# A recurrent attention stage with one decay scan a pair and its inverse summed on TensorE, and a last stage worked in quads

## The chip, the core and the metric

The kernel runs on one core of a Trainium2 chip. The metric is device time in microseconds (us), from one launch to its end. The core's engines are TensorE (PE, with its weight loads as PEld), VectorE (DVE), ScalarE (ACT), GpSimd (POOL) and SyncE (SP), which here only issues DMAs. TensorE's clock is granted at one of two levels, 2.4 GHz (1.00 in the profile) or 1.2 GHz (0.50).

## What is computed

A linear recurrent attention over 4 batches x 8 heads, 768 steps, 40 dimensions a head, then a top-2 mixture of experts (8 experts, 3072 tokens, 320 -> 1024 -> 320), then a feed-forward layer with the gate h * tanh(softplus(h)). All inputs are float32.

```python
for t in range(S):
    y[:, :, t] = np.einsum('bhd,bhde->bhe', rt, state)
    Sa = np.einsum('bhde,bhe->bhd', state, at)
    state_decay = state * wt[:, :, None, :] - np.einsum('bhd,bhe->bhde', Sa, bt)
    state = state_decay + np.einsum('bhd,bhe->bhde', vt, kt)
...
for e in range(E):
    for k in range(2):
        mask = top2[:, k] == e
        h = np.maximum(x[mask] @ w1[e], 0.0)
        out[mask] += top2_w[mask, k, None] * (h @ w2[e])
...
h = x @ w_in
sp = np.where(h > 20.0, h, np.log1p(np.exp(np.minimum(h, 20.0))))
return ((h * np.tanh(sp)) @ w_out).astype(np.float32)
```

## The kernel before

Four stages follow each other: attention, routing (`route`), the expert tiles (`experts`), and the last feed-forward layer (`mish_ffn`). The change touches the first and the last.

**Attention.** The 768 steps are cut into 12 chunks (NC) of 64 (C), two halves of 6 chunks (HC). The 32 heads are 16 pairs; a group holds two pairs (i = 0, 1), so there are 8 groups (GR). A pair's two heads lie in partitions 0 to 63 and 64 to 127. Within a chunk the recurrence is solved in closed form: the decays are folded into `a`, `b` and `k`; N and T are the strictly triangular products of `a` with `b`, and the inverse of one minus N is built by squaring: `npow` and `tpow` hold the powers 2, 4, 8, 16 (steps n2 to n16, t2 to t8), and `wb` the running sum (steps w2 to w16). Steps L, E and F refine it once in float32. Other steps are M, G, K, B, V (products that don't need the state), and UT, ST, H, J, Y, X, which form the output of a half. Each of these steps, called "wide", is one call of `wide(tok, g)` on TensorE: 24 or 48 small matmuls into one of three PSUM buffers `wide0` to `wide2`, which ScalarE or VectorE (`take`) empties. `BY_ACT` names those that ScalarE empties. The step's buffer is reused three steps later, so TensorE waits for that.

The state itself passes from chunk to chunk in a chain of "hops" in PSUM tile `chain`: `u` (ScalarE copies it to `un`), `s` (VectorE updates `st`) and `r` (VectorE adds to `rhs`), 34 hops a group.

What sets the order is the written table `ORDER`. Every engine walks through it once an iteration, 10 iterations (GR + 2) in all: in one iteration stand the wide steps of group g, the chain of group g - 1 with the first-half output steps, and the second-half output steps of group g - 2. `p0` and `p1` are VectorE's `make_decays` for the next group. SP loads the inputs of the next group at fixed places of the table (decays and `a` at its start, `kbv` and `r` when G1 is filled), and POOL scales `a`, `k`, `b` with the decays (`scale_a`, `scale_kb`), for which N0 of the next group waits.

The decays of a chunk are cumulative products. Before, each pair takes two scans over 768 columns, one forwards (`dec`) and one backwards (`after`), a ratio `fend` and a reciprocal of 12 columns; the state is carried divided by decays, and `s` adds with a scalar per chunk, `fs` being the scaled old state that VectorE prepares behind each `r`.

Ahead of all this POOL sets the padded input tiles, after which SP may load; VectorE clears tiles and makes masks; ScalarE issues one DMA that zeroes `slots` (9 MB) for the routing stage.

**Last stage** (`mish_ffn`). Its 24 row tiles are worked in 6 groups of 4 (GT); the 16 column blocks of the hidden layer (FT) each take three matmuls of 512 columns over 128, 96 and 96 input rows (`KT`). ScalarE runs exp block by block, then ln and tanh for a whole group at once; VectorE caps and copies each hidden block out of PSUM and multiplies (`gate`) the group before. `rows_out` of a group stands behind the next group's hidden blocks.

## Time and profile before

| | us |
|---|---|
| time, median of 3 runs | 1853.9 (1849.0 to 1856.9) |
| the profiled execution, its own time | 1852.9 |
| its span | 1851.0 |
| attention: TensorE's first matmul, its last | 47.0, 683.2 |
| busy in the span: TensorE, its weight loads | 1526.4, 1211.4 |
| busy in the span: VectorE, ScalarE, POOL | 600.5, 469.2, 296.9 |
| mean granted clock of TensorE | 0.864 |

The profile is of one execution. Its views are: the page (shares, 40 slices, chain, groups), the groups of instructions by line, the waits (who waited for whom), the DMA queues, the timeline, and stretches ("windows") with the busy time of each engine and the granted clock. "Idle ... <- X" names what ended an engine's idle time; "issue" is time in which it waited for nothing that the profile shows. An engine's busy time is not its bound: what counts is what ends last in each stage.

### The profile page before, as it was taken

To read this page: it belongs to the slowest core of one execution; us is meant where nothing else is said; L and a number is where in the kernel's file an instruction comes from. 1 tells how busy PE (TensorE), PEld (TensorE's weight loads), DVE (VectorE), ACT (ScalarE), POOL (GpSimd) and SP (SyncE) were. 2 spreads that over 40 slices of the span, in tenths; PEclk is the share of its full clock that TensorE was granted. 3 is DMA by queue.
4 is the path that set the end of the run, shared out by engine and by line. 5 is a ranking of instruction groups with operands and counts; after the bars stand their busy time and mean duration, and the time that the engine had idled before them with its cause. 6 is when DMAs were issued, how large, how long until landed. Compare 5 with 4: busy or idle time off the path is not lost. (4 is left out here: it accounts for less than half of the span.)

```text
span 1851.0 us, 52932 instructions
## 1 busy us (share of the span) xinstructions
PE 1526.4 (82%) x23913; PEld 1211.4 (65%) x23913; DVE 600.5 (32%) x1176; ACT 469.2 (25%) x845; POOL 296.9 (16%) x273
## 2 busy tenths in 40 slices
PE   0778777777778769009999999999959999999999
PEld 0777677777777659008888888888834555565556
DVE  5554545545454311300000000000015625526251
ACT  0322323223233211001111111111103635243340
POOL 6413212132221000450000000000031100100000
PEclk9667877787777855559999999999979999999999
DMA  7412111221110019236555555555351100100000
GB/s 260 134 36 69 52 52 54 72 77 52 52 52 25 10 37 295 78 140 211 170 170 175 177 178 178 177 175 174 117 160 49 29 23 28 29 22 0 15 7 22
DMA packets 98652, 177.36 MB, mean 96 GB/s; under 512 B 37280, under 2 KB 66720, under 8 KB 97152
## 3 DMA queue, kind: packets, MB, share of 16 engines
q1 hardware_dynamic: 84128, 140.23, 24.8%
q0 software_dynamic: 7248, 24.75, 4.0%
q10 hardware_dynamic: 7056, 9.01, 1.4%
q8 instruction: 191, 3.13, 0.7%
q14 instruction: 29, 0.24, 0.0%
HBM read 140.20 MB, written 33.75 MB: 94 GB/s over the span
## 5 line engine op out<-in xcount | busy, mean ns | idle before, releaser
L1071 PE MATMUL mpH<-mxT,win 96*128 96x512 f32 (+1 forms) x576 | 253.4, 596 | 2.2 <-ACT mxT L1107 2.2
L948 PE MATMUL pY<-down,hT 128*128 x880 | 245.9, 433 | 0.0
L929 PEld LDWEIGHTS pH<-exT,up 128*128 128x128 f32 x1760 | 207.8, 194 | 15.0 <-DMA up_rest<-in_moe_w 4.9
L929 PE MATMUL pH<-exT,up 128*128 128x128 f32 x1760 | 208.3, 277 | 5.9 <-DMA up_rest<-in_moe_w 4.4
L984 DVE COPY ys<-pY 128x320 f32<-128x320 f32 x55 | 27.1, 492 | 570.6 <-PE pY L948 570.6
L1080 PE MATMUL mpY<-wout,h 128*128 128x320 f32 x768 | 207.5, 432 | 0.0
L948 PEld LDWEIGHTS pY<-down,hT 128*128 128x128 f32 x880 | 163.0, 190 | 61.2
L1071 PEld LDWEIGHTS mpH<-mxT,win 96*128 96x128 f32 (+1 forms) x576 | 108.4, 191 | 133.3 <-issue 129.8
L1080 PEld LDWEIGHTS mpY<-wout,h 128*128 128x128 f32 x768 | 145.6, 190 | 60.5 <-issue 0.5
L975 ACT ACTIVATE hT<-pH 128x512 f32<-128x512 f32 x110 | 59.7, 594 | 422.6 <-PE pH L934 422.6
L1115 ACT ACTIVATE act_in<-act_in 128x512 f32<-128x512 f32 x96 | 59.9, 629 | 243.1 <-DVE act_in L1157 243.1
L908 POOL DMA_DIRECT2D results<-ys x55 | 29.8, 541 | 509.4 <-DVE ys L984 509.4
L482 ACT ACTIVATE npow<-wide 128x768 bf16<-128x768 f32 x80 | 64.8, 810 | 160.5 <-PE wide L298 135.4
L1157 DVE TENSOR_SCALAR act_in<-mpH 128x512 f32<-128x512 f32 x96 | 66.3, 691 | 83.7 <-PE mpH L1071 82.4
L918 PE MATMUL pX<-ident,xs 128*128 128x128 f32 x110 | 24.4, 304 | 74.6 <-DMA xs<-slots 74.6
L1050 POOL DMA_INDIRECT rows<-results,pos x48 | 46.7, 973 | 221.5 <-DVE mix L1133 205.8
L268 POOL TENSOR_TENSOR kbvT<-kbvT,after 128x768 f32<-128x768 f32 x32 | 57.4, 1825 | 93.9 <-DMA kbvT<-in_kbv 93.9
L1138 DVE COPY y<-mpY 128x320 f32<-128x320 f32 x24 | 11.8, 492 | 174.5 <-PE mpY L1080 168.3
L1158 DVE COPY h<-mpH 128x512 f32<-128x512 f32 x96 | 65.5, 682 | 0.0
L918 PEld LDWEIGHTS pX<-ident,xs 128*128 128x128 f32 x110 | 11.2, 142 | 81.6 <-DMA xs<-slots 75.1
L934 PE MATMUL pH<-exT,up_rest 64*128 64x128 f32 x880 | 63.9, 285 | 0.0
L449 PE MATMUL chain<-rhs,w 64*64 64x40 f32 x768 | 50.2, 261 | 16.3 <-DVE rhs L591 14.7
(173 smaller groups left out, 2304.3 us busy)
## 6 DMA issues: line engine op xcount, KB each, us to landing
up<-in_moe_w SPq DMA_DIRECT2D x55, 1024.0 KB, 5.3
up_rest<-in_moe_w SPq DMA_DIRECT2D x110, 128.0 KB, 5.2
kbvT<-in_kbv SPq DMA_DIRECT2D x32, 360.0 KB
down<-in_moe_w SPq DMA_DIRECT2D x8, 1280.0 KB, 14.2
slots<-zero_row ACTq DMA_DIRECT2D x1, 8800.0 KB, 48.1
xs<-slots SPq DMA_DIRECT2D x55, 160.0 KB, 5.1
results<-ys POOLq DMA_DIRECT2D x55, 160.0 KB, 2.1
wfr<-in_wdec SPq DMA_DIRECT2D x32, 240.0 KB
```

The source lines that it names most:

```text
L268: nc.gpsimd.tensor_tensor(kbvT[i][:, j, :], kbvT[i][:, j, :], after[i][:, ::-1], ALU.mult).then_inc(kb_scaled, 1)
L449: m = pe.matmul(chain[x:x + 64, i, 64:64 + D], w0[b2][x:x + 64, i, cols(c, C)], rhs[b2][x:x + 64, i, c, :], start=(c == 0), stop=True, ski ...
L482: return nc.scalar.activation(out, in_, ACT.Copy, scale=scale)
L929: pe.matmul(pH[t % 2][b][:, c, :], up[t % NU][:, k, f * P:(f + 1) * P], xT[t % 2][:, k, :], start=(c == 0 and k == 0), stop=False, skip_gr ...
L934: m = pe.matmul(pH[t % 2][b][:, c, :], up_rest[t % NU][at, c * P:(c + 1) * P], xT[t % 2][at, 2, :], start=False, stop=True, skip_group_che ...
L948: m = pe.matmul(pY[t % 2][:, 0:D], hT[t % 2][:, j, :], down[:, bass.ds(e, 1), j, :].rearrange("q n d -> q (n d)"), start=(j == 0), stop=(j ...
L975: nc.scalar.activation(hT[t % 2][:, b * HT:(b + 1) * HT, :], pH[t % 2][b][:], ACT.Relu).then_inc(h_copied[b], 1)
L1071: m = pe.matmul(pH[n % 4][:], win[0:kn, k, f * P:(f + 1) * P], xT[g % 2][0:kn, k, :], start=(k == 0), stop=(k == 2))
L1080: m = pe.matmul(pY[t % 2][:, 0:D], h[g % 2][:, f, j * P:(j + 1) * P], wout[:, f, :], start=(f == 0), stop=(f == FT - 1))
L1115: nc.scalar.activation(act_in[g % 2][:, f, :], act_in[g % 2][:, f, :], ACT.Exp).then_inc(exped, 1)
L1157: nc.vector.tensor_scalar(act_in[g % 2][:, f, :], pH[n % 4][:], 20.0, None, ALU.min).then_inc(h_min, 1)
L1158: nc.vector.tensor_copy(h[g % 2][:, f, :], pH[n % 4][:]).then_inc(h_used, 1)
```

## The change

In attention:
- `make_decays` is one scan over 12 x 65 columns (`dec`, with the decay at the end of a chunk in column 64) and one reciprocal of 768 columns (`rec`), which scales `k` and `b`.
- The state is carried unscaled: an `s` hop adds (`total`) and then multiplies by the chunk's decay (`past`); `fs` is gone.
- For the odd pair (i = 1) the powers, the running sum, L, E and F alternate between straight and swapped halves (`turned`, `flips`), so that both pairs together use all four quarters; ST and J likewise, for which `r` of the odd pair is loaded a second time (`rTo`).
- The running sum is formed in PSUM: each `w` step gets 24 more matmuls with the identity (`plus=wb`); ScalarE then copies w2, w4, w8, VectorE copies w16.
- E adds the identity on VectorE, and POOL subtracts it from `n32` ahead of time (before, POOL prepared `wm` behind w16).
- `ORDER` is a new table.
- At the start VectorE sets `wtok`; SP loads the decays behind that, `r` and `v` next, then `a` and `kbv`, each behind its own memset; the zeroing of `slots` waits for `kbv` and uses rows of 640 bytes.

In the last stage a quad (four column blocks) is the unit: eight matmuls over 128 rows, then four over 64 rows that stand alternately in the lower and upper half (`win_rest`); exp, ln and tanh follow in each quad, `act_in` has three buffers, and the turn of a row tile and `rows_out` of one row tile stand behind each quad.

```diff
-ORDER = """N0 u UT1 s N1 ST1 r T0 u H1 T1 s M0 r J1 u Y1 s M1 r n2_0 u t2_0 K s n2_1 p0 r t2_1 B u X1 p1 s G0 r n4_0 t4_0 u
-G1 s n4_1 t4_1 w2_0 r V0 u w2_1 n8_0 s t8_0 w4_0 r V1 u n8_1 t8_1 s w4_1 UT0 r n16_0 w8_0 u ST0 n16_1 s w8_1 H0 r
+ORDER = """N0 u UT1 s N1 r T0 ST1 u H1 t2_0 s T1 J1 r Y1 u n2_0 s n2_1 w2_0 r M1 u n4_0 w2_1 s M0 w4_0 r p0 B u t2_1 V1
+s n4_1 t4_0 r G0 u UT0 s t8_0 w4_1 r n8_0 u V0 n16_0 p1 t4_1 s K ST0 r G1 u w8_0 n8_1 s t8_1 r u w8_1 n16_1
...
-BY_ACT = ("n2", "n4", "n8", "n16", "t2", "t4", "t8", "K", "B", "V", "L", "UT", "ST", "X")
+BY_ACT = ("n2", "n4", "n8", "n16", "t2", "t4", "t8", "w2", "w4", "w8", "K", "B", "V", "L", "UT", "ST", "X")
...
+        def turned(i, x, flip):
+
+            return 64 - x if flip and i else x
...
-            sp.wait_ge(pads_set, 1)
+            sp.wait_ge(w_pads, 1)
             load_decays(0)
-            load_a(0)
-            load_kbv(0)
             load_r(0)
             load_v(0)
+            sp.wait_ge(pads_set, 1)
+            load_a(0)
+            sp.wait_ge(pads_set, 2)
+            load_kbv(0)
+            sp.wait_ge(pads_set, 3)
...
-            def square(b, g, half, out, left, right):
+            def square(half, out, left, right, flips, plus=None):
+
                 for c in range(HC):
                     k = half * HC + c
                     for i, h, e, x in cells():
-                        m = pe.matmul(out[x:x + 64, i, cols(c, C)], left[x:x + 64, i, cols(k, C)], right[x:x + 64, i, cols(k, C)],
-                                      start=True, stop=True)
+                        q, z = turned(i, x, flips[0]), turned(i, x, flips[1])
+                        m = pe.matmul(out[z:z + 64, i, cols(c, C)], left[q:q + 64, i, cols(k, C)], right[q:q + 64, i, cols(k, C)],
+                                      start=True, stop=plus is None)
+                    if plus is not None:
+                        for i, h, e, x in cells():
+                            q, z = turned(i, x, flips[0]), turned(i, x, flips[1])
+                            m = pe.matmul(out[z:z + 64, i, cols(c, C)], identh[q:q + 64, q:q + 64], plus[q:q + 64, i, cols(k, C)],
+                                          start=False, stop=True)
                 return m
...
-                        if p == 1:
-                            m.then_inc(carried, 1)
+                        for i, h, e, x in cells():
+                            r = rTo[b3][x:x + D, cols(k, C)] if i else rT[b3][x:x + D, 0, cols(k, C)]
+                            pe.matmul(out[e:e + D, i, cols(c, C)], sm[x:x + D, i, k, :], r, start=(k in (1, HC)), stop=False, skip_group_check=True)
...
-                after_step(nc.vector.tensor_tensor_scan(after[i][:], wfr[i][:, 1, :], mark_r[:], 0.0, ALU.mult, ALU.add))
-                after_step(nc.vector.tensor_tensor(fend[:, g % 3, i, :], after[i][:, ::-1][:, 0::C], wfr[i][:, 0, 1::C], ALU.mult))
-                after_step(nc.vector.reciprocal(mark[:, 0::C], fend[:, g % 3, i, :]))
-                nc.vector.tensor_tensor_scan(dec[g % 3][i][:], wfr[i][:, 0, :], mark[:], 0.0, ALU.mult, ALU.add).then_inc(decayed, 1)
+                after_step(nc.vector.tensor_tensor_scan(dec[g % 3][:, i].rearrange("q c f -> q (c f)"), wtok[i][:].rearrange("q c f -> q (c f)"),
+                                                        mark[:].rearrange("q c f -> q (c f)"), 0.0, ALU.mult, ALU.add))
+                nc.vector.reciprocal(rec[i][:], dec[g % 3][:, i, :, 1:C + 1]).then_inc(decayed, 1)
...
-                    nc.vector.scalar_tensor_tensor(st[:, 1, c + 1, :], chain[:, 1, 128:128 + D], fend[:, g % 3, 1, c + 1:c + 2], fs[:, 1, :],
-                                                   ALU.mult, ALU.add).then_inc(state_ready, 1)
+                    nc.vector.tensor_tensor(total[:], chain[:, :, 128:128 + D], st[:, :, c, :], ALU.add).then_inc(summed, 1)
+                    dve.wait_ge(summed, (NC - 2) * g + c)
+                    nc.vector.tensor_tensor(st[:, :, c + 1, :], total[:], past, ALU.mult).then_inc(state_ready, 1)
...
-                for k, (k0, kn) in enumerate(KT):
-                    m = pe.matmul(pH[n % 4][:], win[0:kn, k, f * P:(f + 1) * P], xT[g % 2][0:kn, k, :], start=(k == 0), stop=(k == 2))
-                m.then_inc(h_done, 1)
...
+                for f in range(GT * q, GT * q + GT):
+                    wait(pe, h_used, g * FT + f - 3)
+                    for k in range(2):
+                        pe.matmul(pH[f % 4][:], win[:, k, f * P:(f + 1) * P], xT[g % 2][:, k, :], start=(k == 0), stop=False)
+                for f in range(GT * q, GT * q + GT):
+                    at = slice(f % 2 * REST, (f % 2 + 1) * REST)
+                    pe.matmul(pH[f % 4][:], win_rest[at, f // 2 * P:(f // 2 + 1) * P], xT[g % 2][at, 2, :],
+                              start=False, stop=True).then_inc(h_done, 1)
...
+                for late in ((), (0,), (1,), (2, 3))[n] if n < GT else (n,):
+                    gate(late)
```

Three places of the instruction order follow. First VectorE in attention, around the decays of pair 0 of the next group (`p0`). `mT` is step M, `rhs` an `r` hop, `st` an `s` hop. Before:

```order
L555 TENSOR_TENSOR mT<-wide0,mask_u 128x2x384
L591 TENSOR_TENSOR rhs0<-chain,rhs0 128x2x40
L593 TENSOR_TENSOR fs<-st,fend 128x80
L599 SCALAR_TENSOR_TENSOR st<-chain,fend,fs 128x40
L601 SCALAR_TENSOR_TENSOR st<-chain,fend,fs 128x40
L581 SCALAR_TENSOR_TENSOR after0<-wfr0,mark_r 128x768
L582 TENSOR_TENSOR fend<-after0,wfr0 128x12
L583 RECIPROCAL mark<-fend 128x12
L584 SCALAR_TENSOR_TENSOR dec2_0<-wfr0,mark 128x768
```

And after the change:

```order
L572 TENSOR_TENSOR mT<-wide0,mask_u 128x2x384
L605 TENSOR_TENSOR rhs0<-chain,rhs0 128x2x40
L596 SCALAR_TENSOR_TENSOR dec2<-wtok0,mark 128x780
L598 RECIPROCAL rec0<-dec2 128x768
L611 TENSOR_TENSOR total<-chain,st 128x80
L613 TENSOR_TENSOR st<-total,dec0 128x2x40
L605 TENSOR_TENSOR rhs0<-chain,rhs0 128x2x40
L572 TENSOR_TENSOR gT1<-wide1,mask_u 128x2x384
```

The decays stood behind an `s` hop's state update and ahead of an `r` hop's addition; they now stand behind an addition and ahead of a state update.

Second TensorE in the last stage, a turn, hidden blocks (`mpH`) and output rows (`mpY`). Before:

```order
L1071 MATMUL mpH0<-mxT1,win 128x512 x3
L1071 MATMUL mpH1<-mxT1,win 128x512 x3
L1071 MATMUL mpH2<-mxT1,win 128x512 x3
L1071 MATMUL mpH3<-mxT1,win 128x512 x3
L1060 MATMUL mpX1<-ident,mix1 128x128
L1060 MATMUL mpX1<-ident,mix1 96x128 x2
L1080 MATMUL mpY0<-wout,h0 128x320 x16
L1080 MATMUL mpY1<-wout,h0 128x320 x16
```

And after:

```order
L1095 MATMUL mpH0<-mxT1,win 128x512 x2
L1095 MATMUL mpH1<-mxT1,win 128x512 x2
L1095 MATMUL mpH2<-mxT1,win 128x512 x2
L1095 MATMUL mpH3<-mxT1,win 128x512 x2
L1098 MATMUL mpH0<-mxT1,win_rest 128x512
L1098 MATMUL mpH1<-mxT1,win_rest 128x512
L1098 MATMUL mpH2<-mxT1,win_rest 128x512
L1098 MATMUL mpH3<-mxT1,win_rest 128x512
L1083 MATMUL mpX0<-ident,mix0 128x128 x3
L1108 MATMUL mpY0<-wout,h0 128x320 x16
```

A block had three matmuls in a row; now four blocks have two each and their third ones stand together, and one row tile's output follows each quad.

Third ScalarE in the last stage, at the end of a group before:

```order
L1115 ACTIVATE act_in<-act_in 128x512 x4
L1106 ACTIVATE mxT<-mpX 128x128
L1107 ACTIVATE mxT<-mpX 96x2x128
L1120 ACT_TABLE_LOAD
L1120 ACTIVATE act_in<-act_in 128x2048 x4
L1123 ACT_TABLE_LOAD
L1123 ACTIVATE act_in<-act_in 128x2048 x4
```

And in every quad after:

```order
L1145 ACTIVATE act_in<-act_in 128x512 x4
L1137 ACTIVATE mxT<-mpX 128x3x128
L1149 ACT_TABLE_LOAD
L1149 ACTIVATE act_in<-act_in 128x2048
L1151 ACT_TABLE_LOAD
L1151 ACTIVATE act_in<-act_in 128x2048
```

Two table loads a group of 16 blocks have become two a quad of four.

## Rows read from the trace of the kernel before

**Rows 1.** Stretches, us: busy (count) PE, PEld, DVE, ACT, POOL; clock, DMA.

```profile
101.00:560.00 459.00, 350.58 (x13716) 333.17 (x13716) 239.39 (x453) 138.17 (x249) 115.61 (x72) 0.76 0.20 58
...
1388.00:1851.00 463.00, 458.57 (x1399) 259.06 (x1397) 208.35 (x352) 171.43 (x196) 31.47 (x32) 1.00 0.07 23
```

**Rows 2.** Waits of PE, 47 to 690 us: us in total, times, longest.

```profile
PE wide L298 <- issue: 32.0, 17, 5.0
PE chain L437 <- DVE st L601: 21.4, 27, 3.2
PE chain L449 <- DVE rhs L591: 14.7, 28, 1.2
...
PE wide L328 <- issue: 0.2, 1, 0.2
```

**Rows 3.** DMA queues, 110 to 560 us, then 580 to 638: packets, MB, share.

```profile
q8 instruction: 106, 1.74, 1.6%
...
q8 instruction: 15, 0.25, 1.9%
```

**Rows 4.** Timeline of TensorE, 286 to 297 us: start us, us, engine, line, operation.

```profile
289.48 0.55 PE L298 MATMUL wide<-wb,npow 64*64 64x64 bf16 x24
289.86 0.55 PE L298 MATMUL wide<-npow,tpow 64*64 64x64 bf16 x24
...
295.51 0.32 PE L298 MATMUL wide<-wb,npow 64*64 64x64 bf16 x5 [3.96 <-issue]
```

**Rows 5.** Groups by line and form: busy us, mean ns of one, idle before.

```profile
L407 PE MATMUL wide<-rT,sm 40*40 40x64 f32 x704 | 36.1, 284 | 0.8 <-issue 0.8
...
L298 PE MATMUL wide<-w,n 64*64 64x64 f32 x768 | 26.9, 226 | 0.0
...
L398 PE MATMUL wide<-rT,unT 40*64 40x64 f32 x768 | 22.0, 264 | 10.2 <-issue 10.2
```

**Rows 6.** Timeline of all engines, 0 to 60 us.

```profile
15.36 3.77 SPq L179 DMA_DIRECT2D wfr<-in_wdec  x4
...
26.77 1.76 DVE L581 TENSOR_TENSOR_SCAN after<-wfr,mark_r 128x768 f32<-128x768 f32 x1 [17.37 <-DMA wfr<-in_wdec]
...
34.38 1.76 DVE L584 TENSOR_TENSOR_SCAN dec<-wfr,mark 128x768 f32<-128x768 f32 x1
...
38.14 7.53 POOL L268 TENSOR_TENSOR kbvT<-kbvT,after 128x768 f32<-128x768 f32 x4
...
47.04 2.84 PE L320 MATMUL wide<-kbvT,aT 40*64 40x64 f32 x96 [47.04 <-DVE mask_un L621]
```

**Rows 7.** Groups by line and form: VectorE's two reciprocals.

```profile
L583 DVE RECIPROCAL mark<-fend 128x12 f32<-128x12 f32 x16 | 3.7, 230 | 0.6
...
L814 DVE RECIPROCAL gates<-gap 128x24 f32<-128x24 f32 x1 | 0.3, 303 | 0.0
```

**Rows 8.** The chain that ended last, in the last stage: start us, us.

```profile
1506.88 10.31 PE mpH L1071 x24
1517.19 0.33 PE mpX L1060 x3
```

**Rows 9.** Timeline of TensorE in the expert stage, 1000 to 1014 us.

```profile
1002.46 3.73 PE L929 MATMUL pH<-exT,up 128*128 128x128 f32 x32
1006.12 1.16 PE L934 MATMUL pH<-exT,up_rest 64*128 64x128 f32 x16
1007.22 0.44 PE L918 MATMUL pX<-ident,xs 128*128 128x128 f32 x2
```

**Rows 10.** Groups by line and form in the last stage: VectorE's, then ScalarE's.

```profile
L1157 DVE TENSOR_SCALAR act_in<-mpH 128x512 f32<-128x512 f32 x96 | 66.3, 691 | 83.7 <-PE mpH L1071 82.4
...
L1115 ACT ACTIVATE act_in<-act_in 128x512 f32<-128x512 f32 x96 | 59.9, 629 | 243.1 <-DVE act_in L1157 243.1
...
L1120 ACT ACTIVATE act_in<-act_in 128x2048 f32<-128x2048 f32 x24 | 43.9, 1897 | 0.1
...
L1120 ACT ACT_TABLE_LOAD x6 | 7.7, 1283 | 0.1
```

More of the change, by code:

```diff
@@ L112, in attention @@
         rT = [sb(f"rT{b}", [P, 2, S]) for b in range(3)]
+        rTo = [sb(f"rTo{b}", [P, S]) for b in range(3)]
         vtok = [sb(f"vtok{b}", [P, 2, NC, D]) for b in range(2)]
@@ L194, in load_r @@
                         sp.dma_start(rT[g % 3][64 * h:64 * h + D, i, :], rt[2 * g + i, h]).then_inc(r_loaded, 16)
+                for h in range(2):
+                    sp.dma_start(rTo[g % 3][64 * (1 - h):64 * (1 - h) + D, :], rt[2 * g + 1, h]).then_inc(r_loaded, 16)
             def load_v(g):
@@ L350, in wide @@
                     left, right = (tpow, npow) if kind[0] == "n" else (npow, tpow)
-                    m = square(b2, g, half, out, left[at_], right[at_])
+                    m = square(half, out, left[at_], right[at_], {2: (0, 0), 4: (0, 1), 8: (1, 0), 16: (0, 1)}[p])
                 elif kind[0] == "w":
@@ L358, in wide @@
                         taken(pe, f"w{p // 2}_{half}", g)
-                    m = square(b2, g, half, out, npow[(p.bit_length() + 1) % 2], wb)
+                    m = square(half, out, npow[(p.bit_length() + 1) % 2], wb, (0, 1) if p in (2, 8) else (1, 0), plus=wb)
                 elif kind == "L":
@@ L364, in wide @@
                         for i, h, e, x in cells():
-                            m = pe.matmul(out[x:x + 64, i, cols(c, C)], wb[x:x + 64, i, cols(k, C)], identh[x:x + 64, x:x + 64], start=True, stop=True)
+                            z = turned(i, x, 1)
+                            m = pe.matmul(out[z:z + 64, i, cols(c, C)], wb[x:x + 64, i, cols(k, C)], identh[x:x + 64, x:x + 64], start=True, stop=True)
                 elif kind == "E":
                     taken(pe, f"w16_{half}", g)
-                    m = square(b2, g, half, out, n32, w0[b2])
+                    pe.wait_ge(less, 2 * g + half + 1)
+                    m = square(half, out, n32, w0[b2], (0, 1))
                 elif kind == "F":
@@ L371, in wide @@
                     taken(pe, f"E{half}", g)
-                    m = square(b2, g, half, out, npow[1], tpow[1])
+                    m = square(half, out, npow[1], tpow[1], (1, 0))
                 elif kind == "UT":
@@ L391, in wide @@
                         for i, h, e, x in cells():
-                            m = pe.matmul(out[e:e + D, i, cols(c, D)], st[e:e + D, i, k, :], ident[e:e + D, e:e + D], start=True, stop=True)
+                            m = pe.matmul(out[x:x + D, i, cols(c, D)], st[e:e + D, i, k, :], ident[e:e + D, e:e + D], start=True, stop=True)
                 elif kind == "H":
@@ L993, in mish_ffn @@
     G = N // P // GT
+    FQ = FT // GT
+    REST = D - 2 * P
     with ExitStack() as ctx:
@@ L1058, in turn, with hidden @@
                 wait(pe, copied, t - 1)
-                for k, (k0, kn) in enumerate(KT):
-                    m = pe.transpose(pX[t % 2][0:kn, k, :], mix[t % 2][:, k0:k0 + kn], ident[:])
+                for k in range(3):
+                    m = pe.transpose(pX[t % 2][:, k, :], mix[t % 2][:, k * P:(k + 1) * P], ident[:])
                 m.then_inc(turned, 1)
-            def hidden(g, f):
-                if f == 0:
+            def hidden(n):
+                g, q = divmod(n, FQ)
+                if q == 0:
@@ L1080, in rows_out @@
+            def rows_out(t, fs):
+                g, j = divmod(t, GT)
+                if fs.start == 0:
+                    wait(pe, y_copied, t - 1)
+                for f in fs:
+                    if j < 2 and f % GT == 0:
+                        pe.wait_ge(gated, g * FT + f + GT)
                     m = pe.matmul(pY[t % 2][:, 0:D], h[g % 2][:, f, j * P:(j + 1) * P], wout[:, f, :], start=(f == 0), stop=(f == FT - 1))
-                m.then_inc(y_done, 1)
+                if fs.stop == FT:
+                    m.then_inc(y_done, 1)
@@ L1083, in _ @@
             for t in range(GT):
                 turn(t)
-            for g in range(G):
-                for f in range(FT):
-                    hidden(g, f)
-                    if f % 4 == 3 and g + 1 < G:
-                        turn((g + 1) * GT + f // 4)
-                if g == 1:
-                    pe.wait_ge(wout_loaded, 16)
-                if g > 0:
-                    for j in range(GT):
-                        rows_out(g - 1, j)
-            for j in range(GT):
-                rows_out(G - 1, j)
+            for n in range(G * FQ):
+                hidden(n)
+                if n + GT < G * GT:
+                    turn(n + GT)
+                if n == GT:
+                    pe.wait_ge(wout_loaded, 16)
+                if n >= GT:
+                    rows_out(n - GT, range(FT))
@@ L1098, in _ @@
+            first = (G - 1) * GT
+            for fs in (range(FT - GT), range(FT - GT, FT)):
+                for t in (first, first + 1):
+                    rows_out(t, fs)
+            for t in (first + 2, first + 3):
+                rows_out(t, range(FT))
         @block.scalar
```

241 lines of the change are left out of this document (110 added, 131 removed).

## The prediction

> **What bounds the kernel now.** I read the profile in this order: stretches of the span with their granted clock, what TensorE waits for, the DMA queues, then single stretches of the timeline.
>
> The stretches say which stage is bound by what. In the last stage, from 1388 us on, TensorE is busy 458.6 of 463 us at clock 1.00 [rows 1]: what it has to stream is the time. In the middle of attention, 101 to 560 us, it is busy 350.6 of 459 us at a mean clock of 0.76, which is 1.2 GHz for half of the time and 2.4 for the other half [rows 1]; the other 108 us are waits. The largest are put down to "issue", TensorE waiting for nothing that the profile shows: thirteen such rows from the first to the last, 91.7 us together. Waits for VectorE come behind: 21.4 us for `st` and 14.7 us for `rhs` [rows 2].
>
> "Issue" is the supply of instructions. Between 110 and 560 us the instruction queue brings 106 packets of 16.4 KB, one per 4.25 us [rows 3]. In about that stretch TensorE executes 2 x 13716 instructions [rows 1], so a packet holds some 254 of them. Where no group's inputs are loaded (580 to 638 us) it is still one packet per 3.87 us [rows 3]. And TensorE stops inside one helper call in which nothing is waited for: 3.96 us before five matmuls of a square, while 24 such matmuls take 0.38 us at full clock (289.48 to 289.86) [rows 4]. So in attention an instruction costs what its share of a packet costs, whatever it computes, unless it streams longer than that.
>
> **The change part by part**, against the profiled execution (1852.93 us, span 1851.0; the median of the three runs is 1.0 us above it).
>
> *Inverse summed on TensorE.* Each of the eight `w` steps of a group gets 24 identity matmuls: 8 x 8 x 24 = 1536, with their weight loads 3072 instructions, 12.1 packets, at 3.87 us: +47 us. Bounds: at 24 in 0.38 us with the supply free, +24 us; at 4.25 us a packet, +51 us. I take the quiet packet, since the bursts of input loads don't multiply. The additions that VectorE loses are not on the path; the copies go to ScalarE, which idles in attention.
> The Trainium skill ("Runtime: NRT & Kernel Launch", Instruction fetch mechanics) says that fetching is hidden, since instructions are dispatched more slowly than the blocks are filled. The stops of 3.96 us within a call speak against it here. By it the sum would have +24 us for this step.
>
> *Odd pair on swapped halves.* Before, steps J (L407) and E (L298 on `w`, `n`, f32) use only two of the four quarters of the array: J costs 36.1/704 = 51 ns a matmul record, E 26.9/768 = 35 ns, while the same form on all four quarters costs 22.0/768 = 28.6 ns [rows 5]. Now both use all four: 704 x 22.7 = 16 us and 768 x 6.4 = 5 us, together -21 us (bounds: nothing, where the supply paces them anyway, and -21). The bf16 squares stream 64 columns in 0.38/24 = 16 ns at full clock [rows 4], under the supply's 3.87/128 = 30 ns a record, so four quarters give them nothing.
>
> *One decay scan a pair.* The two scans, the ratio and the small reciprocal (9.4 us for two pairs, 26.77 to 36.14 [rows 6]) become one scan of 1.8 us and a reciprocal of 768 elements a row. No row shows such a one. 12 elements take 230 ns and 24 take 303 ns [rows 7], 6.1 ns an element: 230 + 756 x 6.1 = 4.8 us. Bounds: an element-wise operation (691 ns for 512 [rows 10]) gives 1.0 us; 303/24 for each element gives 9.7 us. I take 4.8, on the slope of the only two rows. The block is then 6.6 us, which cannot be interrupted, twice an iteration; behind it on VectorE stands the state update, for which the next `r` hop waits.
> The cover: from `rhs` to that `r` hop the new order puts B, a `u` hop, t2_1, V1, the `s` hop, n4_1 and t4_0, some 240 records, 8 us at 33 ns (4.25/128). The second block has n8_0, u, V0, n16_0, t4_1, s, K and ST0, 280 records, 9 us. Block and state update (7.2 us) fit in both: no cost, as long as the reciprocal stays under about 5.6 us.
>
> *Unscaled state.* An `s` hop has two dependent operations where two independent ones stood, and the rescaling behind `r` is gone. Only where the chain runs alone, eleven chunks at the end, does it count: +1 us.
>
> *New order.* VectorE has 144 fewer rows, and dependent steps stand further apart. TensorE's two largest waits for VectorE sum to 36 us [rows 2]; I take not quite a quarter off: -8 us; bounds -25 and +25, since the order can as well put two late producers in a row. G1 moves behind the second block, and SP issues the loads of `kbv` and `r` behind G1. There remain some 820 records, 27 us, for the load (1.4 MB; 9 us is my estimate) and POOL's scaling (7.5 us [rows 6]): hidden, with 10 us to spare.
>
> *Start.* Before: SP issues the first load at 15.36 us, behind all of POOL's memsets, VectorE starts at 26.77, has both pairs at 36.14, and the masks, slowed while POOL scales, take until 47.04 [rows 6]. Now SP waits for two memsets of VectorE, about 2.7 us, and the zeroing of `slots` no longer competes. The decays land before VectorE has done its other memsets (about 10 us); two blocks end at 23.2; the same 10.9 us for masks give 34. So -13 us. Bounds by the reciprocal: 1.0 us gives -20, 9.7 us -3. The zeroing now runs behind the first loads, over POOL's and VectorE's preparation and the first steps of TensorE; before, it reached some 10 us into them as well: 0.
>
> *Last stage.* Four column blocks cost 10.31 us in 24 records of 0.43 us [rows 8]. Now 16 full records (6.87 us) and four pairs of half-height records. The expert stage shows such pairs: sixteen records of 128 columns take 1.10 us (1006.12 to 1007.22 [rows 9]), where eight full ones take 0.93 (3.73 us for 32). So they do run side by side, and going in and out costs 0.17 us. 6.87 + 4 x 0.43 + 0.17 = 8.76 us: -1.55 x 24 = -37 us.
> Something is late behind it. While no output rows are due, TensorE needs 9.1 us a quad (8.76 and 0.33 for the transposes [rows 8]). ScalarE needs 4 x 0.63, a copy of about 0.5, 2 x 1.90 and now two table loads of 1.28 a quad [rows 10]: 9.4 us. Its first quad is done 12.3 us after the first hidden block (VectorE's 3 x 1.38 + 0.69, then one exp, the copy, and both loads and long operations), its fourth at 12.3 + 3 x 9.4 = 40.5; VectorE then gates it (4 x 0.69) and only then mixes the rows that the turn behind the fifth quad needs (about 1.2 us, an estimate), at 44.5. TensorE is there at 4 x 9.1 + 0.9 = 37.3: +7 us, once (bounds 0 and +10). Later a quad has 17 us of TensorE, and VectorE's loop (12.3 + 2.8 + 1.2 + 0.5 = 16.8) fits. Net -30 us.
>
> **Sum:** +47 - 21 + 0 + 1 - 8 - 13 - 30 = -24 us: 1852.9 - 24 = 1829 us.
>
> **The rivals.**
> *A, the supply does not pace it.* Then the identities cost 24 us instead of 47, and the bf16 squares gain from four quarters at the low clock, where a record of 64 columns takes 53 ns and two at a time make 27 a record: a few ns of each of some 4200, about 10 us. 1829 - 23 - 10 = 1796 us. For it: at the low clock TensorE hardly stops. Against: 92 us of stops. It is what the Trainium skill's section on instruction fetch (in "Runtime: NRT & Kernel Launch") would lead to. Its chance is 0.25.
> *B, the reciprocal is uncovered (slower).* Place: the blocks on VectorE ahead of the state update. Price at 9.7 us: a block and update of 12.1 us against covers of 8 and 9 us, 7 us an iteration, 7 iterations, 49 us, and 10 us at the start: 1888 us. It turns the whole to slower from a reciprocal of about 8 us on. Against: the slope of [rows 7]. Chance 0.1.
> The Trainium skill ("VectorE: DVE Perf Modes", the 8-slice pipeline) has the divide repeat 8 times an element; at its 0.96 GHz that is an estimate of 6.4 us, which costs about 9 us here by the same working.
> *C, the gains of attention don't come.* J and E are paced by the supply already (+21), a packet costs 4.25 us (+4) and the new order wins no waits (+8): 1862 us. Chance 0.17.
> *D, the change doesn't do what it says:* records of 512 columns don't pair in the last stage, +37: 1866 us. Against: [rows 9]. Chance 0.04.
> The forecast has 0.44.
>
> **How the numbers follow.** A measurement can tell about 0.5%, 9 us, from no change. Under 1844.6 us lie most of the forecast (0.37), A, and a little of C: 0.65. Within lie the rest of the forecast and most of C: 0.18. Above lie B, D and the tail of C: 0.17. The range 1790 to 1866 holds the forecast, A and most of C and leaves out B.
>
> **What would show it.** TensorE's first matmul at 34 us; RECIPROCAL of 768 elements at 4.8 us; 203 instruction packets, an iteration of attention 1 to 3 us longer than before; J and E under 30 ns a record; quads of 8.76 us; one wait of some 7 us for `mix` behind the fifth quad; a last stage of about 435 us. Wrong would be: fewer "issue" waits with as many packets (A), `st` waits of several us twice an iteration (B), a long wait of N0 for POOL's scaling, or rows in the last stage of 10.3 us a quad (D).

## The result, and the profile after

The changed kernel takes 1870.4 us (median of 5 runs, 1863.6 to 1873.0) where the kernel before takes 1853.9 (1849.0 to 1856.9). The ratio is 1.0088, with a 95% interval of [1.0062, 1.0114]: 16 us slower. The forecast was 1829 us, with a range of 1790 to 1866: the change went the other way, and the time lies outside the range. The profiled execution has a span of 1869.0 us, 18.0 more than before.

The starts and ends of TensorE's work in the two traces (us) give the place:

| | before | after | changed by | forecast |
|---|---|---|---|---|
| first matmul | 47.04 | 36.86 | -10.2 | -13 |
| attention, first to last matmul | 636.2 | 692.9 | +56.7 | +19 |
| routing and experts, up to VectorE's last copy of results | 673.1 | 673.0 | -0.2 | 0 |
| last stage, first hidden block to last matmul | 465.1 | 437.7 | -27.4 | -30 |

The start and the last stage came nearly as forecast. Attention lost three times what was forecast.

The profile's page of the changed kernel: the clock granted to TensorE in 40 slices, and the DMA queues (packets, MB, share).

```profile
PEclk9996666657765766555999999999997999999999
...
q10 hardware_dynamic: 14096, 9.01, 1.6%
q8 instruction: 203, 3.33, 0.8%
```

The 203 instruction packets are the number forecast. Next, TensorE's waits in the changed kernel from 30 to 700 us (engine, tile and line, what was waited for: us in total, times, longest), the answer to [rows 2]:

```profile
PE wide L310 <- issue: 53.6, 36, 5.9
...
PE wide L336 <- ACT xr L495: 27.8, 5, 6.2
PE chain L450 <- DVE st L613: 16.5, 23, 1.6
PE wide L336 <- issue: 15.6, 11, 2.7
...
PE chain L462 <- DVE rhs L605: 5.2, 14, 1.1
```

The waits for VectorE fell from 21.4 and 14.7 us to 16.5 and 5.2, and "issue" rose (all its rows: 135 us, where 92 stood). The row of `xr` was not in the trace of before at all: step N (L336 in the changed kernel) waits five times, up to 6.2 us, for ScalarE's copy into `xr`, the attention output on its way to memory.

One of the five, in the timeline of all engines around 427 us (start us, us, engine, line, operation; in brackets the idle time ahead):

```profile
426.07 0.43 PE L462 MATMUL chain<-rhs,w 64*64 64x40 f32 x8
426.59 0.83 SPq L204 DMA_DIRECT2D vtok<-in_vtok  x2
427.47 5.22 SPq L210 DMA_DIRECT2D x_by_pair<-xr  x4
431.13 0.63 ACT L495 ACTIVATE xr<-wide 128x240 f32<-128x240 f32 x2 [8.69 <-DMA x_by_pair<-xr]
...
431.81 1.56 PE L336 MATMUL wide<-kbvT,aT 40*64 40x64 f32 x48 [5.31 <-ACT xr L495]
```

Read it from the end. TensorE's N0 cannot start before 431.81, because it reuses the PSUM buffer of X0, and ScalarE copies X0 out only from 431.13 on. ScalarE was idle for 8.69 us, since it copies into `xr` only when the earlier stores from it have landed. SP issued the last of these at 427.47, behind the load of `v`, and that load stands behind a wait for the last `u` hop, 426.07. So the last hop of an iteration, a load, a store, its landing, a copy and the first step of the next iteration became one chain. Before, the store stood ahead of the loads of `kbv`.

### The profile page after: what moved, and what is told of

Read it like the earlier page. It is cut to its first block and busy times, and to the rows that moved or that the text cites. A ratio compares the mean times of both kernels' runs of the same rounds, so it can differ in the third digit from the quotient of the medians.

```text
span 1869.0 us, 55904 instructions
## 1 busy us (share of the span) xinstructions
PE 1492.0 (80%) x25449; PEld 1180.2 (63%) x25449; DVE 607.3 (32%) x1041; ACT 554.8 (30%) x905; POOL 284.3 (15%) x268
## 5 line engine op out<-in xcount | busy, mean ns | idle before, releaser
L1095 PE MATMUL mpH<-mxT,win 128*128 128x512 f32 x384 | 173.3, 605 | 4.9 <-ACT mxT L1137 4.7
L1095 PEld LDWEIGHTS mpH<-mxT,win 128*128 128x128 f32 x384 | 74.1, 194 | 92.2 <-issue 82.8
L1175 DVE TENSOR_TENSOR h<-h,act_in 128x512 f32<-128x512 f32 x96 | 59.9, 686 | 142.8 <-ACT act_in L1151 142.7
L310 PE MATMUL wide<-wb,npow 64*64 64x64 bf16 x1536 | 60.3, 234 | 26.3 <-issue 23.0
L598 DVE RECIPROCAL rec<-dec 128x768 f32<-128x768 f32 x16 | 79.2, 4953 | 0.5
L336 PE MATMUL wide<-kbvT,aT 40*64 40x64 f32 x768 | 24.3, 300 | 64.7 <-DVE mask_un L635 36.9
L275 POOL TENSOR_TENSOR kbvT<-kbvT,rec 128x768 f32<-128x768 f32 x32 | 57.4, 1826 | 93.8 <-DMA kbvT<-in_kbv 93.8
L495 ACT ACTIVATE un<-chain 128x80 f32<-128x80 f32 x96 | 22.9, 238 | 163.9 <-PE chain L462 163.7
```

The source lines that it names most:

```text
L275: nc.gpsimd.tensor_tensor(kbvT[i][:, j, :], kbvT[i][:, j, :], rec[i][:].rearrange("q c f -> q (c f)"), ALU.mult).then_inc(kb_scaled, 1)
L310: m = pe.matmul(out[z:z + 64, i, cols(c, C)], left[q:q + 64, i, cols(k, C)], right[q:q + 64, i, cols(k, C)], start=True, stop=plus is None)
L495: return nc.scalar.activation(out, in_, ACT.Copy, scale=scale)
L598: nc.vector.reciprocal(rec[i][:], dec[g % 3][:, i, :, 1:C + 1]).then_inc(decayed, 1)
L1095: pe.matmul(pH[f % 4][:], win[:, k, f * P:(f + 1) * P], xT[g % 2][:, k, :], start=(k == 0), stop=False)
L1175: nc.vector.tensor_tensor(at, at, act_in[n % 3][:, f, :], ALU.mult).then_inc(gated, 1)
```

## The experiments

Ratios are to the kernel before, measured beside each, with 95% intervals; 0.1% is 1.85 us. Differences between two kernels are taken between their ratios. Lines in a trace move by one or more with each edit.

**1. The store ahead of the wait.** In the changed kernel the store of the second half goes ahead of the wait for the last hop (not back to its old place ahead of `kbv`, since X1 comes late in the new order):

```diff
                     sp.wait_ge(filled, number["V1", it] + 1)
+                if it >= 2:
+                    store(it - 2, 1)
+                if g < GR:
                     if it >= 1:
                         sp.wait_ge(hopped, it * HOPS)
                     load_v(g)
-                if it >= 2:
-                    store(it - 2, 1)
```

> The changed kernel with one edit: SP issues the store of the second half of x (group it-2) ahead of its wait for the last hop and ahead of the load of v, not behind them. Theory S (the moved store): ScalarE's copy of x for the first half waits for that store to land, and the next N step of TensorE waits for that copy, 27.8 us in five waits of the changed kernel's trace, one for each iteration that both loads and stores. They go: 1870 - 28 = 1842 us, no wait of TensorE on xr over 1 us, an iteration of attention about 5.6 us shorter. Rival I (instruction supply): attention's 57 us come from instructions; packets go on arriving at one per 4.2 us and the waits on xr turn into waits put down to issue: 1862 to 1870 us.

Measured: 0.9960 [0.9925, 0.9994]; the same kernel measured again (experiment 3), 0.9969 [0.9946, 0.9993]. That is 22 to 24 us faster than the changed kernel, and attention takes 668.6 us in the trace instead of 692.9. The row of waits for `xr` is gone. SP's store now follows a copy into `xr` at once (timeline, 400 to 417 us):

```profile
404.94 0.61 ACT L496 ACTIVATE xr<-wide 128x240 f32<-128x240 f32 x2
405.62 1.93 SPq L210 DMA_DIRECT2D x_by_pair<-xr  x2
```

Theory S holds. The other way round, the same edit was made alone in the kernel before:

```diff
-                if it >= 2:
-                    store(it - 2, 1)
...
                     load_v(g)
+                if it >= 2:
+                    store(it - 2, 1)
```

> The kernel before with only SP's store of the second half moved behind the load of v, as in the changed kernel. Theory S: the copy of x for the first half then waits for a store that is issued only behind the last hop, and F1, which reuses its buffer, waits for the copy: five times about 5.6 us, 1854 + 28 = 1882 us. Rival I: the wait is an effect of the new order alone, and here the store has slack: 1854 to 1858 us.

Measured: 1.0094 [1.0059, 1.0129], 17 us slower. Its waits show the new row, in the place where it was expected:

```profile
PE wide L298 <- ACT xr L482: 27.3, 5, 6.0
```

27.3 us of waits cost 17 to 19 us (attention is 19.2 us longer, 655.4). The expectation of 28 took each wait at its full length, but some of it had stood elsewhere before: in the traces TensorE's "issue" waits in attention fell from 91.8 to 84.8 us.

**2. The identities.** The early-store kernel (that of experiment 1) first without them, so that the running sum is left out, and then with all of them at an eighth of their columns, so that most of the sum is left out:

```diff
-m = square(half, out, npow[(p.bit_length() + 1) % 2], wb, (0, 1) if p in (2, 8) else (1, 0), plus=wb)
+m = square(half, out, npow[(p.bit_length() + 1) % 2], wb, (0, 1) if p in (2, 8) else (1, 0))
```

> The previous kernel (early store) without the 1536 identity matmuls of the eight w steps: the sum with the old w is left out of the computation, nothing takes its place. Supply theory of the prediction: 3072 instructions fewer, 12 packets at 3.9 us: 47 us less than the kernel with them. Rival A of the prediction (the supply does not pace it, an instruction costs its streaming): 24 us less. A third: the time is set by waits between engines and the identities stand in their shade, under 15 us less.

Measured: 0.9759 [0.9700, 0.9817]: 37 us less than with them by the ratios, 43 by the medians, 45 in attention's time in the traces (623.4 for 668.6 us). It is the +47 of the forecast, a little less. The two intervals together allow some 12 us either way, so that the 24 of rival A lies at their edge; experiment 6, which does the sum without identities, gains 45 us with 10 either way and leaves it out.

```diff
-m = pe.matmul(out[z:z + 64, i, cols(c, C)], identh[q:q + 64, q:q + 64], plus[q:q + 64, i, cols(k, C)],
+m = pe.matmul(out[z:z + 64, i, c * C:c * C + 8], identh[q:q + 64, q:q + 64], plus[q:q + 64, i, k * C:k * C + 8],
...
```

> The kernel with the early store, with all 1536 identity matmuls in place, each adding 8 of its 64 columns only (the rest of the sum is left out). Supply theory: the instruction count sets the time, 1845 us as with 64 columns. Work theory (rival A): 56 of 64 columns less at 10 to 19 ns a record, about 20 us less, 1825 us or below.

Measured: 0.9951 [0.9923, 0.9978], 2 to 3 us less than with 64 columns, which the intervals cannot tell from none. The pages have the same packets in the kernel with 8 columns, and 12 fewer without the identities:

```profile
q8 instruction: 203, 3.33, 0.7%
```

```profile
q8 instruction: 191, 3.13, 0.7%
```

So an identity costs because it is an instruction, and hardly for what it streams. Where a packet comes each 3.87 us ([rows 3]), twelve are 46 us.

The short identities alone can't tell the supply from a fixed cost of each matmul on TensorE itself: with 8 columns as with 64 an identity starts on average 13.6 ns behind the matmul ahead of it (gaps of 200 ns and more left out). But 1536 times 13.6 ns are 21 us, half of what the identities cost, and without them TensorE's "issue" waits in attention fall from 140.1 to 116.1 us. Experiment 3 is the other half of the argument: there work is taken away and no instruction, and nothing is gained.

The Trainium skill ("Runtime: NRT & Kernel Launch", Instruction fetch mechanics) has fetching hidden behind the dispatch of instructions; in this stage, with 64-column matmuls, these runs speak against it.

**3. Four quarters instead of two.** The early-store kernel, with J as in the kernel before (e5), with the squares, E, F and L in one place (e6), and with both (e14). The core of the edits:

```diff
-            return 64 - x if flip and i else x
+            return x
...
-r = rTo[b3][x:x + D, cols(k, C)] if i else rT[b3][x:x + D, 0, cols(k, C)]
-pe.matmul(out[e:e + D, i, cols(c, C)], sm[x:x + D, i, k, :], r,
+m = pe.matmul(out[e:e + D, i, cols(c, C)], sm[e:e + D, i, k, :], rT[b3][e:e + D, i, cols(k, C)],
...
```

> The kernel with the early store, but step J again on two quarters of TensorE's array, pair 1 first and pair 0 behind it, as in the kernel before (the extra rows of r are still loaded). The prediction's term: 704 records from 28.6 to 51 ns, 16 us more than 1845. If the supply paces J either way, as the small gain of the whole suggests: 0 to 5 us more.

> The kernel with the early store, but every step that the change put on swapped halves except J (the squares n, t, w with their identities, L, E and F) on two quarters again. The prediction's term: E 5 us, bf16 squares nothing: 5 us more. By the record rates in the two traces (bf16 squares 26 and 14 ns a record where the clock is low) up to 30 us more. If the supply paces all: 0.

Measured: 0.9979 [0.9943, 1.0014] and 0.9936 [0.9909, 0.9963]; against 0.9960 that is 3.5 us more and 4.4 us less, both inside the intervals. To settle it, both edits together and the kernel without them were measured side by side:

> The kernel with the early store, with J and the squares, E, F and L all on two quarters of the array: the change without its swapped halves. The prediction's terms J and E are 21 us: 1866 us. From the two single runs (J +4, the squares -5, both within their intervals): 1840 to 1850 us, no difference from the same kernel on four quarters in this call.

> The kernel with the early store again, as the mate of the one on two quarters in this call: 1845 us.

Measured: 0.9964 [0.9942, 0.9986] on two quarters, 0.9969 [0.9946, 0.9993] on four (medians 1844.1 and 1844.3 us). Together the swapped halves are worth nothing; 21 us lie outside what the two intervals allow (about 6 us either way). Yet the edit does what it says. Busy time of the engines from 101 to 560 us, as in [rows 1], first on two quarters, then on four:

```profile
101.00:560.00 459.00, 361.11 (x14139) 346.04 (x14136) 235.80 (x314) 159.39 (x269) 106.37 (x68) 0.73 0.17 50
```

```profile
101.00:560.00 459.00, 337.33 (x14200) 316.57 (x14204) 233.88 (x315) 160.24 (x273) 106.52 (x68) 0.67 0.18 53
```

TensorE gets through as many matmuls in the stretch (14139 and 14200). On four quarters it is busy 23.8 us less for them, and this at a lower mean clock; it stands idle for what it saved. "Issue" waits of the whole stage are 143 us where the other kernel has 128. It looks as if a faster step only reached the next missing instruction earlier; the runs show the idle time, not its cause. (Over the whole of attention the two profiled executions are 10 us apart, 669.8 us on four quarters and 680.0 on two, but the profiled execution on two quarters was the slowest of its twelve, 1858.4 us; the ratios show no difference.)

**4. The order.** The early-store kernel with the table `ORDER` of the kernel before, then the kernel before with the new table (its store of the second half moved ahead of the wait for the last hop, as in experiment 1, because X1 comes late in the new order):

```diff
-ORDER = """N0 u UT1 s N1 r T0 ST1 u H1 t2_0 s T1 J1 r Y1 u n2_0 s n2_1 w2_0 r M1 u n4_0 w2_1 s M0 w4_0 r p0 B u t2_1 V1
+ORDER = """N0 u UT1 s N1 ST1 r T0 u H1 T1 s M0 r J1 u Y1 s M1 r n2_0 u t2_0 K s n2_1 p0 r t2_1 B u X1 p1 s G0 r n4_0 t4_0 u
...
```

> The kernel with the early store in the order of steps of the kernel before. The prediction has the new order at 8 us (bounds -25 and +25): 8 us more than 1845. Rival: the new order gains nothing or loses, since dependent steps of a square now wait in it less but producers are late in a row: 1845 or less.

> The kernel before in the new order of steps, with the store of x's second half issued ahead of the wait for the last hop (in the new order that half is ready only late in the iteration). The prediction gives the new order 8 us, bounds -25 and +25: 1852 - 8 = 1844 us. If the order is worth in the kernel before what it is worth in the changed one (37 to 49 us), 1805 to 1815 us. If it serves only to cover the new, longer decay block, 1852 us or more.

Measured: 1.0187 [1.0141, 1.0234] for the old order in the changed kernel, 42 us more than the new; 0.9951 [0.9933, 0.9969] for the new order in the kernel before, 9 us less than before, the 8 us of the forecast. The two numbers differ because the decay block has changed. With the old order, the early-store kernel waits for `st`, at most 5.7 us at a time:

```profile
PE chain L451 <- DVE st L614: 46.7, 32, 5.7
```

The old order has a block right ahead of an `r` hop (`p0`) and right ahead of an `s` hop (`p1`), whose additions VectorE then makes late. In the new order VectorE can start a block as soon as it has done an `r` hop's addition, and a `u` hop and three wide steps or more (B, t2_1 and V1; n8_0, V0, n16_0 and t4_1) come ahead of the `s` hop whose state it must update next. The trace tells the block from the unscaled state, whose two dependent operations are new as well: with the old order a scan or reciprocal of the decays ran during 16 of TensorE's waits for `st` and `rhs`, 44.4 us together; in the early-store kernel this happens in two waits, 0.4 us. How much of the cover is used up shows with the reciprocal computed twice:

```diff
+                after_step(nc.vector.reciprocal(rec[i][:], dec[g % 3][:, i, :, 1:C + 1]))
                 nc.vector.reciprocal(rec[i][:], dec[g % 3][:, i, :, 1:C + 1]).then_inc(decayed, 1)
```

> The kernel with the early store, with each reciprocal of the decays computed twice, one behind the other: a block on VectorE takes 1.8 + 2 x 4.95 = 11.7 us and not 6.8. By the prediction's covers of 8 and 9 us (its rival B: 59 us at 9.7 us more than it took for the reciprocal) it loses 5 us at each of the 14 blocks behind the first group and 10 us at the start: about 1845 + 50 = 1895 us, with waits of TensorE for st of 3 to 5 us twice an iteration. If the covers are much longer than counted: 1855 us, the start alone.

Measured: 1.0231 [1.0192, 1.0270], 1895.5 us, 50 us more. The first matmul comes at 46.73, and the wait for `st` is back:

```profile
PE chain L451 <- DVE st L615: 70.6, 27, 6.3
```

20.3 us stood in that row with one reciprocal. Twelve of the waits, two in each of six iterations, are 4.1 to 6.3 us long, 61.8 us together, and a decay block runs in each: there the second reciprocal was charged in full. The cover is real and hardly longer than the block. Of the 14 x 4.95 = 69 us that were added behind the start, 40 us (ratios) to 49 us (traces) came through, since other waits became shorter. (The expectation's own terms, 14 x 5 and 10 at the start, make 80 us and not the 50 that it gives.)

**5. The last stage alone,** put into the kernel before (its function `mish_ffn` exchanged whole):

```diff
-            for g in range(G):
-                for f in range(FT):
-                    hidden(g, f)
...
+            for n in range(G * FQ):
+                hidden(n)
...
```

> The kernel before with the changed kernel's last stage alone. The two traces give the last stage 484.1 us before and 455.6 us now, from the first gather's queue to the last matmul: 1854 - 28 = 1826 us. Rival: the stage gained only because something ahead of it (code, loads) was already there, then 1840 us or more.

Measured: 0.9857 [0.9800, 0.9915], 26 us less by the ratios, 31 by the medians (1822.8 us). It does not depend on what stands ahead of it.

**6. What beats both.** The early-store kernel with the additions on VectorE again. An addition takes both pairs at once and needs the product in the partitions of the old sum, so n, t and w stay on two quarters, which experiment 3 says is free:

```diff
-BY_ACT = ("n2", "n4", "n8", "n16", "t2", "t4", "t8", "w2", "w4", "w8", "K", "B", "V", "L", "UT", "ST", "X")
+BY_ACT = ("n2", "n4", "n8", "n16", "t2", "t4", "t8", "K", "B", "V", "L", "UT", "ST", "X")
...
-m = square(half, out, npow[(p.bit_length() + 1) % 2], wb, (0, 1) if p in (2, 8) else (1, 0), plus=wb)
+m = square(half, out, npow[(p.bit_length() + 1) % 2], wb, (0, 0))
...
+                elif kind in ("w2", "w4", "w8"):
+                    m = nc.vector.tensor_tensor(wb[:, :, at_], t, wb[:, :, at_], ALU.add)
+                elif kind == "w16":
+                    m = nc.vector.tensor_tensor(w0[b2][:, :, at_], t, wb[:, :, at_], ALU.add)
```

> The kernel with the early store and with the sums of the w steps on VectorE again instead of 1536 identity matmuls; n, t and w squares are on two quarters, E, F, L and J on four. Without the sums at all it took 1802 us. Supply theory: the additions are hidden, 1800 to 1810 us. Rival: VectorE's 64 additions and the ScalarE copies that they replace shift work onto the engine that the chain waits for: 1815 to 1830 us.

Measured: 0.9717 [0.9679, 0.9755], 1796.9 us: 52 us faster than the kernel before, 69 faster than the changed one. VectorE is busy 282.2 us from 101 to 560 us instead of 238.6, and it costs nothing measurable against the kernel without any sum (0.9759).

The gain can be put together from parts that have been measured: the new order in the kernel before (0.9951), the last stage alone (1.43% less) and the earlier start (10 us, 0.55%) make 0.9753. The new decays, the unscaled state and J and E on four quarters, which this kernel has besides, are then worth 7 us together, and the intervals allow some 13 either way.

The same with the old order:

> The kernel with early store and sums on VectorE (1797 us) in the order of steps of the kernel before. With identities the old order cost 37 us, in waits for st of up to 5.7 us. If that is the decay block on VectorE, which the old order does not cover, it costs as much here or more, since VectorE has the additions as well: 1835 to 1845 us. If it is the identities that the old order cannot place: within 10 us of 1797.

Measured: 0.9981 [0.9959, 1.0002], 49 us more, with 43.8 us of waits during which a decay block ran. So it is the decay block that the old order fails to cover, and not the identities.

Two small edits on top (SP then waits for the third of GpSimd's clearings only ahead of loading `a` of the next group):

```diff
+                if n == GT - 1:
+                    take_turned(n + GT)
                 for f in range(GT):
                     act.wait_ge(h_min, n * GT + f + 1)
...
-            for b in (1, 2):
-                m = nc.gpsimd.memset(aT[b][:], 0.0)
-            m.then_inc(pads_set, 1)
...
+                if g == 0:
+                    for b in (1, 2):
+                        m = nc.gpsimd.memset(aT[b][:], 0.0)
+                    m.then_inc(pads_set, 1)
```

> The kernel with early store and sums on VectorE (1797 us) and two small edits: GpSimd clears aT of the groups 1 and 2 behind its first rounding and not while VectorE makes the masks (first matmul from 36.9 to about 34 us), and ScalarE takes the eighth turned rows ahead of the fourth quad's exps (TensorE's stop of 4.1 us in the last stage to about 1.5). Together 5 us less, 1792 us; if the first matmul's gain is lost in attention, 1795 us.

Measured: 0.9703 [0.9668, 0.9737], 1790.3 us, 3 us less than without, inside the interval. The first matmul moved to 34.24 as meant. The other edit only traded waits: its 4.7 us are gone, and 5.4 stand in their place. TensorE's waits in the last stage, first of the changed kernel (the one that this builds on has the same 4.7), then of this one:

```profile
PE mpH L1095 <- ACT mxT L1137: 4.7, 2, 4.1
```

```profile
PE mpX L1087 <- DVE mix L1169: 3.5, 1, 3.5
PE mpH L1099 <- ACT mxT L1141: 1.9, 2, 1.3
```

## Why the prediction was wrong, point by point

**The step that failed first: the moved store.** The prediction's part on the new order follows SP's loads of `kbv` and `r` past G1 and finds them hidden, and it stops there. The same part of the diff moves `store(it-2, 1)` behind the load of `v`, whose wait is the last hop of the iteration. That store is what ScalarE waits for before it takes X0, and X0's buffer is what N0 wants. The term "new order" put this at nothing without a word; it costs 22 to 24 us in the changed kernel (experiment 1) and 17 in the one before. The code shows who waits for `x_stored`, so the chain could have been forecast.

**The second: J and E on four quarters, -21 us.** The rates behind it are right. J runs as forecast, in the timeline of the changed kernel, two records of each pair in turn:

```profile
685.28 0.33 PE L425 MATMUL wide<-rT,sm 40*40 40x64 f32 x2
685.31 0.32 PE L425 MATMUL wide<-rTo,sm 40*40 40x64 f32 x2
685.38 0.35 PE L425 MATMUL wide<-rT,sm 40*40 40x64 f32 x2
685.42 0.32 PE L425 MATMUL wide<-rTo,sm 40*40 40x64 f32 x2
685.48 0.35 PE L425 MATMUL wide<-rT,sm 40*40 40x64 f32 x2
```

Four records start in 0.10 us, 26 ns each, under the 30 that the prediction asked for. But the gain was measured at nothing (e14 and e15). The prediction had said itself that in attention an instruction costs its share of a packet, and then compared step by step: 51 ns is more than the supply's 30, so J must gain. The comparison that counts is over the whole stretch. In [rows 1] 27432 instructions are some 107 packets, and at 3.87 us ([rows 3]) these take 415 of the 459 us. A step that streams more slowly than it is supplied leaves instructions waiting, and the next, faster one uses them up. That last sentence is argued from the totals; what the runs show is that 24 us of busy time turned into 24 us of idle time. The remark that four quarters would give the bf16 squares nothing was right for the time and wrong for the rate: they start every 16 to 17 ns at the low clock, where it was 27, and every 13 at the full clock, where it was 16 to 17 (means over attention, gaps of 200 ns and more left out).

**Identities, +47:** 37 to 45 measured. A packet count times the quiet spacing gave the right size; twelve packets at 37 to 45 us are 3.1 to 3.75 us each, so 3.87 was slightly dear, and the bounds (24, 51) held it. Against rival A stand the size (experiments 2 and 6) and the swapped halves that gained nothing (experiment 3); the run with short identities refutes only a price by the column. That the stops put down to "issue" are missing instructions is inferred from packet counts; no view shows it directly.

**Decay blocks, 0:** the reciprocal of 768 elements takes 4953 ns, where the slope of [rows 7] gave 4.8 us. Groups of VectorE by line and form:

```profile
L598 DVE RECIPROCAL rec<-dec 128x768 f32<-128x768 f32 x16 | 79.2, 4953 | 0.5
...
L596 DVE TENSOR_TENSOR_SCAN dec<-wtok,mark 128x780 f32<-128x780 f32 x16 | 28.3, 1770 | 0.0
```

The cover was also right: with one reciprocal the wait for `st` stays where it was (20.3 us for 21.4), with two it costs 50 us where the prediction's rival B had 59 for about the same length. The Trainium skill ("VectorE: DVE Perf Modes", the 8-slice pipeline) led to an estimate of 6.4 us; the trace has 4.95.

**New order, -8:** -9 in the kernel before. But the entry in the sum hides that in the changed kernel the order carries 42 to 49 us: with the new blocks in the old order the change would have been lost outright. "Decays 0" and "order -8" were one term.

**Unscaled state, +1:** not tried alone. With J and E at 0, the identities, the order and the store account for attention's change as 45 - 9 + 24 = 60 us, against 56.7 in the traces. What is left for the decays and the state, -3, is inside the intervals, as are the 7 us of experiment 6; that the terms add up like this is assumed.

**Start, -13:** -10.2. The working missed 2.7 us of GpSimd's clearing of `aT`, which ran while VectorE made the masks (moved away in e12, it gave 2.6 us back); one mask copy took 4.58 us there (timeline, 10 to 37 us) where a copy of the same kind takes 0.34:

```profile
31.14 4.58 DVE L632 COPY mask_ln<-n 64x384 f32<-64x384 f32 x1
35.64 0.34 DVE L632 COPY eye<-ident 64x384 f32<-64x384 f32 x1
```

**Last stage, -30:** -27.4 from the first hidden block on. The chain that ended last, early and late in the stage of the changed kernel, answers [rows 8]:

```profile
1440.38 7.13 PE mpH L1095 x16
1447.51 1.92 PE mpH L1098 x8
...
1473.24 7.11 PE mpH L1095 x12
```

```profile
1510.96 6.87 PE mpH L1095 x16
1517.83 1.92 PE mpH L1098 x8
1519.74 0.48 PE mpX L1083 x3
1520.22 8.62 PE mpY L1108 x32
```

A late quad takes 6.87 + 1.92 = 8.79 us; 8.76 was forecast. Rival D is refuted by it. The one stop behind the fourth quad is there, but it is 4.1 us and not 7, and it ends with ScalarE's copy `mxT`, which stands behind the exps of the fourth quad. The wait for `mix` that the prediction named is next in the queue: it came up as 3.5 us when the copy was taken earlier (e12).

The sum with what was measured: +43 for the identities, 0 for J and E, 0 for the decays, -9 for the order, -10 for the start, -28 for the last stage and +23 for the store is +19 us, against 16 in the medians and 18 between the traces. Of the 41 us between forecast and result, the store is 23 and J and E are 21; the smaller misses cancel but for 3 us the other way.

The range failed with it. Rival C (1862 us) had the second error in it, and none had the first. An item of the diff that has no price belongs in the range, with the longest wait that it could form.

## What to carry to other kernels

When an entry moves in a queue's list, follow what every entry is waited for by, stores too: a store moved behind a wait is a release of a buffer moved behind that wait. Where instructions set the pace, count them over the whole stretch and don't credit any single step that gets faster; take them away instead, as by leaving additions on an idle engine. A long block that cannot be interrupted and the order that covers it are one edit, and neither has a price of its own.

## What the runs showed of the hardware that was not expected

- 64 x 64 squares in bf16 that alternate over all four quarters of the array start every 16 to 17 ns on average at the low clock and every 13 ns at the full one (27 and 16 to 17 ns on two quarters), and the kernel is no faster for it.
- The same 1536 matmuls cost as much with 8 columns as with 64 (within 3 us of 37 to 45), and they follow each other no faster (13.6 ns either way).
- From 101 to 560 us, with as many matmuls, TensorE was busy 337 us at a mean granted clock of 0.67 on four quarters and 361 us at 0.73 on two: a mix of the levels 1.2 and 2.4 GHz in both.
- A reciprocal of 768 elements a row takes 4953 ns, 2.8 times a scan of 780.
- VectorE's copies of 64 x 384 elements take 0.34 us alone and 1.8 to 1.95 us while GpSimd scales; one took 4.58 us, in which GpSimd ended its scaling and cleared two buffers.
